# Splitting the causal mask of a decay product between its spare rows and an identity product, with constants, loads and two engines' orders rearranged

## Chip, cores and metric

One core of one Trainium2 chip. The metric is the device time of one execution in microseconds, median of several runs. Engines: PE (TensorE; its weight loads are shown apart as PEld), DVE (VectorE), ACT (ScalarE), POOL (GpSimd) and SP (SyncE, which here only issues DMAs).

## What is computed

A gated linear attention (2 batches, 8 heads, 768 steps, head size 40) feeds a dense mixture of four experts and then a gated product layer. All inputs are f32.

```python
for t in range(S):                       # attention
    m_new = np.maximum(f_gate[:, :, t] + m, i_gate[:, :, t])
    f_stab = np.exp(f_gate[:, :, t] + m - m_new); i_stab = np.exp(i_gate[:, :, t] - m_new)
    C = f_stab * C + i_stab * outer(vt, kt); n = f_stab * n + i_stab * kt
    y[:, :, t] = sigmoid(o_gate[:, :, t]) * (C @ qt) / max(abs(n @ qt), 1)
for e in range(4):                       # experts, x is y as 1536 x 320
    out += p[:, e:e+1] * (np.maximum(x @ w1[e], 0) @ w2[e])
result = ((out @ w_a) * (out @ w_b)) @ w_out
```

## The kernel before

**Attention in chunks.** Time is cut into 6 chunks of 128 steps; a chunk of one batch is a *unit*, 12 in all (`NU`), unit u being chunk u // 2 of batch u % 2. Inside a unit the recurrence becomes products: scores (`products`, L1519), times weights exp(log decay), times values (`outputs`, L1562), plus the part from the state (`from_state`, L1531), and an update of the state (`update`, L1545). The log weight of key step s and query step t is a sum of a term of s and a term of t, and minus 1e30 where s > t. `log_weights` makes it on PE for 4 heads at a time (q = 0, 1): first an identity product adds the mask (`identb` times `mask`, bf16, 512 columns, L1507), then the decay product (`dec_l` times `dec_r`, 66 rows, 512 columns, L1508) adds the rest. In `dec_l`, rows 0 to 15 and 32 to 47 hold the key term's high and low halves for the 16 heads, and rows 64 and 65 are ones; in `dec_r`, rows 0 to 63 pick the head and rows 64 and 65 hold the query term. ACT takes exp of both banks (`weights`, L602), DVE multiplies with the scores (`weigh`, L1063).

**Start.** POOL builds `identf`, `pick`, `ones`, `mask`, `identb` and parts of `dec_l` one after the other, counting them in `pool_const` and `mask_ready`. DVE clears the `qk` buffers and part of `dec_l`, then `first_logs` scans the gates of chunks 0 and 1 (from L1153 on) and makes the halves of the query terms, `lhi` (L1142) and `llo` (L1145). SP and ACT send these rows into `dec_r` by DMA, PE turns them into unit 0's log weights. Meanwhile a second scan (L1165) gives `m` for the rest, a DMA brings it back into another layout (`m_r`), and `rest_logs` makes the terms of chunks 2 to 5, which `load_dec_l` and `load_rows` bring by DMA into `dec_l` and `dec_r`. PE runs dummy products (`keep_busy`, L1481) while it has nothing else. SP's issues are written in a fixed order, each behind waits on semaphores.

**The layers.** 56 *groups* (`NG`): 8 plain ones, groups 8 to 31 for experts and 32 to 55 for the gated layer. From group 8 on a group has 7 products of 4 matmuls with 384 columns (L1619 to L1622) in two PSUM banks A and B, in a form with 7 instead of 8 block products. ACT and DVE combine them: ACT copies `keep_p1`, `keep_u2`, `keep_w` (L737, L745, L751), DVE makes `c11`, `c22`, `c12` (L1229, L1236, L1243), ACT rounds the result to the high half `hh` (L729), DVE makes the low half `hl` (L1214, L1220). Between a group's products PE does the second layer of the group before (L1700, 320 columns). Product 1 of a group waits till `c12` of the group before has left bank B (`b_free`), product 2 till `keep_p1` has left bank A.

**Groups 29, 30, 33 and 34** also turn the result of the layer before for the next (`turn_within`, 4 transposes each, L1472 and L1474): ACT replicates tails (`replicate`, L615), copies the turned tiles (`keep_turned`, L626) and rounds them (`x_high`, L641); DVE makes low halves (`x_low`, L1018, L1019) and differences (`x_sum`, L1038) for groups 32 and 36. New weights go through ACT (`high_a` L692, `high_s` L696), POOL (`low_a` L508, four `sums` L518 to L524, `low_s` L513); `high_s` of a tile can begin when POOL's four sums are done. What ACT and DVE do in these groups is written out by hand in `turning_expert`, `expert_group`, `turning_gated` and `gated_group`; engines work strictly in this order.

## Time and profile before

| what | us |
|---|---|
| median of 3 runs | 609.79 (609.6 to 610.05) |
| the profiled execution's own time | 610.64 |
| its span in the profile | 608.5 |
| PE busy | 599.8 (99%) |
| PE weight loads | 581.7 (96%) |
| DVE / ACT / POOL busy | 358.6 / 290.9 / 179.6 |
| granted TensorE clock, mean | 0.998 |

A timeline row gives start, length, engine, line and operation; a bracket at its end is the engine's idle time before it and what ended that. Ends of PE's matmuls are modelled, so an idle gap on PE shows best in the distance between starts.

### The profile page before, as it was taken

The numbers are of one execution on the slowest core, as the hardware profiler recorded it, in microseconds if no ns is written. First come the engines' busy times: TensorE is split into PE (matmuls) and PEld (weight loads), VectorE is DVE, ScalarE is ACT, GpSimd is POOL, SyncE is SP. The second block draws the span as 40 slices with busy tenths as digits, with TensorE's granted clock in tenths as the row PEclk, the third lists the DMA queues.
The fourth block names the chain that finished last, engine by engine and source line by source line (L and its number), as shares of the span: only waits on it lengthen the run. The fifth ranks groups of instructions, "written<-read, shape, count | busy, mean of one in ns | idle before, by whom it ended". The sixth has DMA issues, their size and how long they took to land.

```text
span 608.5 us, 10953 instructions
## 1 busy us (share of the span) xinstructions
PE 599.8 (99%) x4001; PEld 581.7 (96%) x4001; DVE 358.6 (59%) x706; ACT 290.9 (48%) x618; POOL 179.6 (30%) x246
## 2 busy tenths in 40 slices
PE   8999999999999999999999999999999999999997
PEld 7788999999999999999999999999899999999996
DVE  7767974454473444543535545477796665666555
ACT  5778745324443444443444434746744543444332
POOL 4466430015330134300334001332325521553000
PEclk9999999999999999999999999999999999999999
DMA  4756541003312021410022200112102410120011
GB/s 131 223 197 180 166 126 49 12 1 69 97 39 61 1 46 30 129 40 23 9 61 87 57 12 0 42 40 80 53 12 46 108 57 12 45 47 1 5 62 65
DMA packets 21028, 38.38 MB, mean 63 GB/s; under 512 B 3520, under 2 KB 11280, under 8 KB 20976
## 3 DMA queue, kind: packets, MB, share of 16 engines
q1 hardware_dynamic: 19040, 35.02, 20.4%
q10 hardware_dynamic: 1936, 2.67, 1.3%
q8 instruction: 32, 0.52, 0.4%
q14 instruction: 20, 0.16, 0.1%
HBM read 26.42 MB, written 1.97 MB: 47 GB/s over the span
## 4 chain that ended last, share of the span: by engine, by line
PE 92%; DVE 4%; DMA 1%; issue 1%; ACT 1%; SPq 0%; DVEq 0%; ACTq 0%
PE PS L1700 37%; PE PS L1619 12%; PE PS L1622 12%; PE PS L1620 11%; PE PS L1621 11%; PE PS L1562 2%; PE PS L1519 1%; PE PS L1531 1%; DMA dec_l<-alo_r 1%; PE PS L1472 1%; PE PS L1474 1%; PE PS L1507 1%; PE PS L1508 1%; PE PS L1545 0%; DMA dec_r<-llo 0%
## 5 line engine op out<-in xcount | busy, mean ns | idle before, releaser
L1700 PE MATMUL PS<-w2h,hh 128*128 128x320 f32 x528 | 164.9, 312 | 0.1
L1700 PE MATMUL PS<-w2l,hh 128*128 128x320 f32 x528 | 163.4, 309 | 0.0
L1700 PE MATMUL PS<-w2h,hl 128*128 128x320 f32 x528 | 163.2, 309 | 0.0
L1619 PE MATMUL PS<-xop,wop 128*128 128x384 f32 x400 | 138.9, 347 | 1.1 <-ACT p_s L737 0.6
L1622 PE MATMUL PS<-xop,wop 96*128 96x384 f32 x400 | 135.1, 338 | 0.0
L1620 PE MATMUL PS<-xop,wop 128*128 128x384 f32 x400 | 134.8, 337 | 0.0
L1621 PE MATMUL PS<-xop,wop 128*128 128x384 f32 x400 | 134.8, 337 | 0.0
L729 ACT ACTIVATE hh<-c_s 128x384 fp32r<-128x384 f32 x120 | 62.8, 523 | 100.4 <-DVE c_s L1243 27.9
L1700 PEld LDWEIGHTS PS<-w2h,hh 128*128 128x128 f32 x528 | 99.5, 189 | 0.8 <-DVE hl L1220 0.8
L1700 PEld LDWEIGHTS PS<-w2l,hh 128*128 128x128 f32 x528 | 99.7, 189 | 0.0
L1700 PEld LDWEIGHTS PS<-w2h,hl 128*128 128x128 f32 x528 | 99.4, 188 | 0.0
L1236 DVE TENSOR_TENSOR c_s<-PS,w_s 128x384 f32<-128x384 f32 x48 | 26.8, 557 | 99.8 <-ACT w_s L751 68.9
L1619 PEld LDWEIGHTS PS<-xop,wop 128*128 128x128 f32 x400 | 75.1, 188 | 6.9 <-issue 1.4
L1620 PEld LDWEIGHTS PS<-xop,wop 128*128 128x128 f32 x400 | 75.3, 188 | 0.0
L1622 PEld LDWEIGHTS PS<-xop,wop 96*128 96x128 f32 x400 | 75.2, 188 | 0.0
L1621 PEld LDWEIGHTS PS<-xop,wop 128*128 128x128 f32 x400 | 75.1, 188 | 0.0
L1214 DVE SCALAR_TENSOR_TENSOR hl<-PS,hh 128x384 fp32r<-128x384 f32 x56 | 31.1, 556 | 57.8 <-ACT hh L729 57.5
L513 POOL TENSOR_TENSOR wop<-s,wop 128x512 fp32r<-128x512 f32 x24 | 31.1, 1297 | 105.4 <-ACT wop L696 105.4
L729 ACT ACTIVATE hh<-PS 128x384 fp32r<-128x384 f32 x56 | 27.4, 489 | 71.8 <-PE PS L1700 38.2
L1214 DVE SCALAR_TENSOR_TENSOR hl<-c_s,hh 128x384 fp32r<-128x384 f32 x72 | 42.6, 592 | 27.9 <-ACT hh L729 27.9
L751 ACT ACTIVATE w_s<-PS 128x384 f32<-128x384 f32 x48 | 23.5, 490 | 64.3 <-PE PS L1622 64.2
L533 POOL TENSOR_TENSOR t1l<-t,t1h 128x384 fp32r<-128x384 f32 (+1 forms) x7 | 7.3, 1050 | 154.5 <-ACT t1h L703 154.5
(148 smaller groups left out, 811.3 us busy)
## 6 DMA issues: line engine op xcount, KB each, us to landing
s<-in_wt SPq DMA_DIRECT2D x24, 256.0 KB, 3.2
kvo<-in_tok SPq DMA_DIRECT2D x12, 480.0 KB, 3.8
wop<-t1h SPq DMA_DIRECT2D x48, 112.0 KB, 2.2
qk<-in_qk_t SPq DMA_DIRECT2D x24, 160.0 KB
s<-in_w SPq DMA_DIRECT2D x12, 320.0 KB, 3.0
wop<-t1l SPq DMA_DIRECT2D x24, 112.0 KB, 2.2
s<-in_w_out SPq DMA_DIRECT2D x12, 160.0 KB, 2.2
out_y<-acc SPq DMA_DIRECT2D x12, 160.0 KB, 1.9
```

What stands on the lines that cost most here:

```text
L513: nc.gpsimd.tensor_tensor(wop[p][:, 2, 3 * P:7 * P], s1[:, p, :], f32(wop[p][:, 0, 3 * P:7 * P]), ALU.subtract).then_inc(w_lo_s, 1)
L533: nc.gpsimd.tensor_tensor(t1l[:, to], t1[:, of], f32(t1h[:, to]), ALU.subtract).then_inc(t_lo, 1)
L729: nc.scalar.activation(hh[:, home(n, k), :], src, ACT.Relu if n < FIRST else ACT.Copy).then_inc(hh_ready, 1)
L751: nc.scalar.activation(w_s[:, :], PS[:, A_BANK, 0:HT], ACT.Copy).then_inc(w_kept, 1)
L1214: nc.vector.scalar_tensor_tensor(out=hl[:, home(n, k), :], in0=src, scalar=0.0, in1=f32(hh[:, home(n, k), :]), op0=ALU.max, op1=ALU.subtra ...
L1236: nc.vector.tensor_tensor(c22_s[:, :], PS[:, B_BANK, 0:HT], w_s[:, :], ALU.add).then_inc(c22_made, 1)
L1562: last = nc.tensor.matmul(PS[:, out_bank(u), D1 * h:D1 * (h + 1)], pt[b][q][:, p, :], vx[b][:, h, :], start=True, stop=True)
L1619: nc.tensor.matmul(to, ws[0], xs[0], start=opens, stop=False, skip_group_check=True)
L1620: nc.tensor.matmul(to, ws[0], xs[2], start=False, stop=False, skip_group_check=True)
L1621: nc.tensor.matmul(to, ws[2], xs[0], start=False, stop=False, skip_group_check=True)
L1622: return nc.tensor.matmul(to, ws[1][0:96, :], xs[1][0:96, :], start=False, stop=closes, skip_group_check=True)
L1700: got = nc.tensor.matmul(bank, left, (w2l if part == 1 else w2h)[p][:, f, :], start=opens and part == 0, stop=closes and part == 2)
```

## The change

Four things. **Mask**: rows 66 to 127 of `dec_r` now hold minus 1e30 on a diagonal over columns 0 to 61 of each head, and the same rows of `dec_l` a staircase of ones, so that the decay product (now 128 rows) masks these 62 columns itself; the identity product covers only the other 66 (264 columns for 4 heads) and comes second. **Constants**: POOL sets all of `dec_l` (one fill, one select over 768 columns) and clears `qk1`; `first_logs` waits for this select; ACT writes two more pieces per `dec_r`. **Loads**: unit 1's `qk` goes behind the first rows, `dec_l` of chunk 2 (units 4 and 5) ahead of unit 2's `kvo` and unit 3's `qk`; `llo` is made before `li` is reduced. **Orders**: ACT and DVE in groups 29 to 35 (`prepare_early`, which held `high_s` and `high_a` of two tiles, is split into `prepare_parted_sums` and `prepare_parted`).

```diff
@@ POOL, start @@
-            nc.gpsimd.memset(f32(dec_l[64:PICKED, :, :]), 1.0).then_inc(pool_const, 1)
+            nc.gpsimd.memset(f32(dec_l[:, :, :]), 1.0).then_inc(pool_const, 1)
             pool.wait_ge(pool_const, 5)
+            nc.gpsimd.affine_select(out=dec_l[:, :, :], in_=dec_l[:, :, :], compare_op=ALU.is_ge, fill=0.0, base=PICKED - 1,
+                                    pattern=[[0, NC], [1, P]], channel_multiplier=-1).then_inc(pool_const, 1)
...
-            nc.gpsimd.memset(f32(dec_l[0:64, 2:NC, :]), 0.0).then_inc(pool_const, 1)
+            nc.gpsimd.memset(qk[1][:, :, :, :], 0.0).then_inc(pool_const, 1)
@@ ACT, def pick_heads @@
+                for at, of, by in ((0, PICKED, NEG), (STEPS, 0, 0.0)):
+                    cols = STEPS if of else P - STEPS
+                    nc.scalar.activation(dec_r[b][64:P, :, at:at + cols], identf[64:P, of:of + cols].unsqueeze(1).to_broadcast([64, H, cols]),
+                                         ACT.Copy, scale=by).then_inc(picked, 1)
@@ DVE, def logs_of @@
-                nc.vector.tensor_tensor(li, li, lsum, ALU.subtract).then_inc(done, 1)
                 dve.wait_ge(done, n + 6)
                 nc.vector.tensor_tensor(llo, lsum, f32(lhi), ALU.subtract).then_inc(rows_ready, 1)
+                nc.vector.tensor_tensor(li, li, lsum, ALU.subtract).then_inc(done, 1)
@@ DVE, def first_logs @@
-                dve.wait_ge(dve_const, 2)
-                dve.wait_ge(pool_const, 4)
+                dve.wait_ge(dve_const, 1)
+                dve.wait_ge(pool_const, 6)
@@ SP @@
-            sp.wait_ge(qk_zero, 2)
-            load_qk(1)
             load_first_high_row(0)
             load_first_high_row(1)
+            sp.wait_ge(pool_const, 11)
+            load_qk(1)
...
             load_qk(2)
+            load_dec_l(2)
             load_kvo(2)
-            load_qk(3)
-            sp.dma_start(pe_w[:, :, :].rearrange("p e u -> p (e u)"), probs).then_inc(probs_in, 16)
-            load_dec_l(2)
@@ PE, def log_weights @@
-                    nc.tensor.matmul(PS[:, DEC + q, :], identb[:, :], mask[:, :, :].rearrange("s p t -> s (p t)"), start=True, stop=False)
-                    nc.tensor.matmul(PS[:, DEC + q, :], dec_l[0:PICKED, c, :], dec_r[b][0:PICKED, q:H:2, :], start=False, stop=True).then_inc(dec_done, 1)
+                    to = PS[:, DEC + q, :]
+                    nc.tensor.matmul(to, dec_l[:, c, :], dec_r[b][:, q:H:2, :], start=True, stop=False, skip_group_check=True)
+                    nc.tensor.matmul(to.rearrange("s (p t) -> s p t", p=NP)[:, :, STEPS:P], identb[:, :], mask[:, :, :],
+                                     start=False, stop=True, skip_group_check=True).then_inc(dec_done, 1)
@@ PE @@
-            keep_busy(14)
+            keep_busy(13)
             products(0)
-            keep_busy(4)
+            keep_busy(3)
@@ ACT, def turning_expert @@
                 keep_u2(n)
-                if b2 is not None:
-                    x_high(b2, 0)
+                prepare_weights(n)
                 high_c11(n)
                 keep_w(n)
                 keep_turn(n, 1)
                 replicate_late(b1, 3)
                 if b2 is not None:
-                    x_high(b2, 1)
+                    x_high(b2, 0)
                 high_c21(n)
                 keep_turn(n, 2)
                 if b2 is not None:
+                    x_high(b2, 1)
                     x_high(b2, 2)
-                prepare_weights(n)
                 high_c22(n)
@@ ACT, def turning_gated @@
                 replicate_late(b2, 5)
+                prepare_parted_sums(n)
                 keep_w(n)
                 keep_turn(n, 1)
-                prepare_early(n)
-                replicate_late(b1, 3)
                 keep_turn(n, 2)
                 high_product(n, 0)
+                prepare_parted(n)
+                replicate_late(b1, 3)
@@ DVE, def expert_group @@
                 low_relu(n, 2, c22_s[:, :])
+                make_c12(n)
                 if b3 is not None:
                     x_low(b3, 4)
-                make_c12(n)
-                if b3 is not None:
                     x_sum(b3, 3)
@@ DVE, def turning_expert @@
                     x_low(b2, 0)
-                    x_low(b2, 1)
                 low_relu(n, 1, PS[:, A_BANK, 0:HT])
                 make_c22(n)
+                if b2 is not None:
+                    x_low(b2, 1)
@@ DVE, def gated_group @@
-                if b3 is not None:
-                    w2_lows(n - 1)
                 make_c12(n)
@@ DVE, def turning_gated @@
                 make_c22(n)
-                if b1 is not None:
-                    x_low(b1, 0)
                 if b2 is not None:
                     x_low(b2, 2)
                 make_c12(n)
                 low_product(n, 0, c11_s[:, :])
                 make_ab2(n)
                 if b1 is not None:
+                    x_low(b1, 0)
                     x_low(b1, 1)
+                if b2 is not None:
+                    w2_lows(n)
```

Where it shows in the orders of the engines:

POOL at the start of the program, before and then now (`pool_const` counts the constants; 6 is the select on `dec_l`).

```order
L458 MEMSET ones 128x128 [waits pool_const]
L459 MEMSET mask 128x512
L462 AFFINE_SELECT mask<-mask 128x512 [waits mask_ready]
L464 CAST identb<-identf 128x128
L466 MEMSET dec_l 2x768 [waits mask_ready]
L469 MEMSET vx0 128x8 [waits pool_const]
L470 MEMSET state0 128x328
```

```order
L458 MEMSET ones 128x128 [waits pool_const]
L459 MEMSET mask 128x264
L462 AFFINE_SELECT mask<-mask 128x264 [waits mask_ready]
L464 CAST identb<-identf 128x128
L465 MEMSET dec_l 128x768
L468 AFFINE_SELECT dec_l<-dec_l 128x768 [waits pool_const]
L471 MEMSET vx0 128x8
```

What `dec_l` needs is now two instructions over 768 columns and stands ahead of the states; DVE's first scan, which waited for `ones`, now waits for the second of them, as the next two pieces show (DVE, first instructions, before and now).

```order
L1118 MEMSET m 16x1
L1119 MEMSET dec_l 64x256
L1120 MEMSET qk0 128x1024
L1121 MEMSET qk1 128x1024
L1153 SCALAR_TENSOR_TENSOR m<-gate,m 16x256 [waits gates_in,pool_const,dve_const]
```

```order
L1126 MEMSET m 16x1
L1127 MEMSET qk0 128x1024
L1159 SCALAR_TENSOR_TENSOR m<-gate,m 16x256 [waits gates_in,pool_const,dve_const]
```

ACT in group 30 and the start of group 31, before and now (`wop1<-s1 128x384` is `high_a`, `wop1<-s1 128x512` is `high_s` of the same tile, `p1_s` is `keep_p1`).

```order
L745 ACTIVATE u2_s<-PS 128x384 [waits c12_made,prod_done]
L641 ACTIVATE xop0<-raw 128x2x384 [waits prod_done,raw_ready]
L729 ACTIVATE hh<-c11_s 128x384 [waits l2_done,c11_made]
L751 ACTIVATE w_s<-PS 128x384 [waits c22_made,prod_done]
L626 ACTIVATE raw<-PS 128x2x2x128 [waits x_lo,xt_done]
L641 ACTIVATE xop0<-raw 128x2x384 [waits prod_done,raw_ready]
L729 ACTIVATE hh<-PS 128x384 [waits l2_done,prod_done]
L626 ACTIVATE raw<-PS 128x2x2x128 [waits x_lo,xt_done]
L641 ACTIVATE xop0<-raw 128x2x384 [waits prod_done,raw_ready]
L692 ACTIVATE wop1<-s1 128x384 [waits prod_done,w_in1]
L729 ACTIVATE hh<-c22_s 128x384 [waits l2_done,c22_made]
L696 ACTIVATE wop1<-s1 128x512 [waits w_sum]
L729 ACTIVATE hh<-c12_s 128x384 [waits l2_done,c12_made]
L737 ACTIVATE p1_s<-PS 128x384 [waits c11_made,prod_done]
```

```order
L750 ACTIVATE u2_s<-PS 128x384 [waits c12_made,prod_done]
L697 ACTIVATE wop1<-s1 128x384 [waits prod_done,w_in1]
L734 ACTIVATE hh<-c11_s 128x384 [waits l2_done,c11_made]
L756 ACTIVATE w_s<-PS 128x384 [waits c22_made,prod_done]
L631 ACTIVATE raw<-PS 128x2x2x128 [waits x_lo,xt_done]
L646 ACTIVATE xop0<-raw 128x2x384 [waits prod_done,raw_ready]
L734 ACTIVATE hh<-PS 128x384 [waits l2_done,prod_done]
L631 ACTIVATE raw<-PS 128x2x2x128 [waits x_lo,xt_done]
L646 ACTIVATE xop0<-raw 128x2x384 [waits prod_done,raw_ready] x2
L734 ACTIVATE hh<-c22_s 128x384 [waits l2_done,c22_made]
L701 ACTIVATE wop1<-s1 128x512 [waits w_sum]
L734 ACTIVATE hh<-c12_s 128x384 [waits l2_done,c12_made]
L742 ACTIVATE p1_s<-PS 128x384 [waits c11_made,prod_done]
```

`high_a`, which starts POOL's chain, moved from the place ahead of `c22`'s rounding to right behind `u2_s`; `high_s`, which ends it, stayed.

DVE in group 31, before and now (`xop0` is `x_low(2, 4)`).

```order
L1214 SCALAR_TENSOR_TENSOR hl<-PS,hh 128x384 [waits hh_ready]
L1214 SCALAR_TENSOR_TENSOR hl<-c22_s,hh 128x384 [waits hh_ready]
L1018 TENSOR_TENSOR xop0<-raw,xop0 128x384 [waits x_hi]
L1019 TENSOR_TENSOR xop0<-raw,xop0 32x384
L1243 TENSOR_TENSOR c12_s<-PS,u2_s 128x384 [waits u2_kept,prod_done]
```

```order
L1220 SCALAR_TENSOR_TENSOR hl<-PS,hh 128x384 [waits hh_ready]
L1220 SCALAR_TENSOR_TENSOR hl<-c22_s,hh 128x384 [waits hh_ready]
L1249 TENSOR_TENSOR c12_s<-PS,u2_s 128x384 [waits u2_kept,prod_done]
L1026 TENSOR_TENSOR xop0<-raw,xop0 128x384 [waits x_hi]
L1027 TENSOR_TENSOR xop0<-raw,xop0 32x384
```

`c12` no longer stands behind the two instructions of `x_low`.

## Rows read from the trace of the kernel before

**Rows 1.** Who waited for whom, engine PE, whole span: us, times, longest
```profile
PE PS L1507 <- DMA dec_l<-alo_r: 1.0, 1, 1.0
```

**Rows 2.** Chain that ended last, 0 to 90 us: start us, us, what
```profile
3.23 0.63 DVE m L1153
...
7.22 2.39 DMA dec_r<-llo
...
16.99 6.50 DMA dec_l<-alo_r
```

**Rows 3.** Timeline of POOL: start us, us, engine, line, operation, count
```profile
1.17 0.29 POOL L453 TENSOR_SCALAR_AFFINE_SELECT identf<-identf 128x128 f32<-128x128 f32 x1 [0.24 <-POOL identf L451]
...
2.64 0.63 POOL L462 TENSOR_SCALAR_AFFINE_SELECT mask<-mask 128x512 bf16<-128x512 bf16 x1
3.22 0.71 POOL L464 CAST identb<-identf 128x128 bf16<-128x128 f32 x1
3.99 0.73 POOL L466 MEMSET dec_l<- 2x768 f32 x1
```

**Rows 4.** Timeline of DVE, the logs of the later chunks begin
```profile
12.41 0.28 DVE L1125 TENSOR_TENSOR lf_r<-gate_r,m_r 80x128 f32<-80x128 f32 x1
```

**Rows 5.** Timeline of PE, start of the program
```profile
2.08 5.20 PE L1481 MATMUL PS<-ones 128*128 128x128 f32 x28 [2.08 <-POOL ones L458]
...
8.30 1.16 PE L1481 MATMUL PS<-ones 128*128 128x128 f32 x8
```

**Rows 6.** Timeline of PE, log weights of unit 6
```profile
35.44 0.39 PE L1507 MATMUL PS<-mask,identb 128*128 128x512 bf16 x1
...
35.90 0.39 PE L1507 MATMUL PS<-mask,identb 128*128 128x512 bf16 x1
```

**Rows 7.** Timeline of PE weight loads, the same place
```profile
35.43 0.10 PEld L1507 LDWEIGHTS PS<-mask,identb 128*128 128x128 bf16 x1
35.44 0.20 PEld L1508 LDWEIGHTS PS<-dec_r,dec_l 66*128 66x128 f32 x1
```

**Rows 8.** Timeline of DVE, unit 7's numerators
```profile
58.11 0.50 DVE L1099 TENSOR_TENSOR num<-PS,inter_s 128x328 f32<-128x328 f32 x1 [0.48 <-PE PS L1562]
```

**Rows 9.** Windows by group: length, busy PE PEld DVE ACT POOL, clock, DMA
```profile
354.24:364.42 10.18, 10.18 (x66) 10.18 (x65) 4.36 (x9) 3.43 (x7) 0.00 (x0) 1.00 0.06 18
...
398.20:409.24 11.04, 10.48 (x67) 10.21 (x65) 8.77 (x14) 5.62 (x11) 3.05 (x4) 1.00 0.14 33
409.24:419.95 10.71, 10.65 (x66) 10.19 (x65) 9.19 (x17) 5.26 (x13) 3.12 (x5) 1.00 0.40 121
419.95:429.54 9.59, 9.30 (x60) 8.84 (x59) 5.86 (x13) 7.98 (x20) 3.54 (x5) 1.00 0.17 46
429.54:439.26 9.72, 9.58 (x59) 8.74 (x59) 7.57 (x14) 7.04 (x15) 2.41 (x3) 1.00 0.17 44
...
447.18:455.62 8.44, 8.37 (x48) 7.52 (x47) 8.15 (x18) 3.66 (x7) 1.86 (x3) 1.00 0.07 20
455.62:463.29 7.67, 7.67 (x48) 7.56 (x47) 5.20 (x11) 3.46 (x7) 3.00 (x6) 1.00 0.01 2
```

**Rows 10.** Timeline of ACT, groups 30 and 31
```profile
395.56 0.51 ACT L692 ACTIVATE wop<-s 128x384 fp32r<-128x384 f32 x1
...
400.17 0.63 ACT L696 ACTIVATE wop<-s 128x512 fp32r<-128x512 f32 x1 [3.15 <-POOL s L524]
```

**Rows 11.** Timeline of DVE, groups 31, 34 and 35
```profile
408.88 0.55 DVE L1018 TENSOR_TENSOR xop<-raw,xop 128x384 fp32r<-128x384 f32 x1
...
410.04 0.56 DVE L1243 TENSOR_TENSOR c_s<-PS,u_s 128x384 f32<-128x384 f32 x1
...
433.20 0.56 DVE L1229 TENSOR_TENSOR c_s<-PS,p_s 128x384 f32<-128x384 f32 x1 [0.54 <-PE PS L1622]
...
446.26 1.20 DVE L1053 TENSOR_TENSOR w2l<-s,w2h 128x320 fp32r<-128x320 f32 x1
```

**Rows 12.** Timeline of ACT, group 33
```profile
426.40 0.58 ACT L626 ACTIVATE raw<-PS 128x512 f32<-128x512 f32 x1
```

37 lines of the change are left out of this document (18 added, 19 removed).

## The prediction

> **What bounds the kernel now.** I read the page first: PE is busy 599.8 of 608.5 us (the table above), so only what shortens PE's own work, or a place where PE stands, can change the time much. The list of PE's waits names one long one in the attention part, 1.0 us for a DMA into `dec_l` [rows 1]; it is short because ends of matmuls are modelled, so I looked for the rest in the lengths of the groups. In the chain that ended last the reader sees how the start hangs together: DVE's first scan at 3.23, the DMA of the first rows at 7.22 (landed 2.39 later), and the DMA of `dec_l` for chunk 2, which took 6.50 us from 16.99 [rows 2]. In the windows by group a quiet expert group takes 10.18 us and a quiet gated one 7.67, with PE full [rows 9]. Groups 31 and 32 take 11.04 and 10.71, so PE stood 0.86 and 0.53 us in them. Groups 33 and 34 have 28 matmuls of 384 columns, 18 of 320 and 12 of a transpose; by the quiet groups (36 of 320 in one, 18 in the other, so 18 of them make 10.18 - 7.67 = 2.51) and 12 transposes at about 0.11 they should take 7.67 + 1.3 = 9.0, and take 9.59 and 9.72: 0.6 and 0.7 lost. Group 36 takes 8.44, 0.77 lost. Together about 3.5 us of standing, and the change rearranges just these groups.
>
> **The change, part by part.**
>
> *Mask products.* Each of 12 units has two identity products of 512 columns, now 264. Start to start, an identity product and its decay product take 35.90 - 35.44 = 0.46 us for 1024 columns [rows 6], so 248 columns are 0.11 us, 0.22 per unit, if nothing else decides. But the first product of each pair is now the decay product, whose f32 weights take 0.20 us to load against 0.10 for the bf16 identity [rows 7], and this load stands right behind a wait, while `dec_l`'s used to lie under the identity's columns. That can give back 0.10 per unit at one exposed load, 0.20 at two. I take 0.10 saved per unit (0 to 0.22), since for one of the two loads 264 columns of the pair before are there to cover it. The Trainium skill (TensorE: Matmul & The Clock Gate, LDWEIGHTS and Weight-path perf modes) says that a load goes by its columns at 1.2 GHz, 107 ns for 128, and that only types other than f32 load faster. By it a streamed 264 columns would just cover a load, and a unit would save some 0.1 us more; by the same rule the swap of a fast first load for a slow one speaks against the change. Rows 7 agree that f32 loads take twice as long as bf16 ones.
>
> *Which units count.* Units 0 to 2 wait for rows, exp and logs, so nothing there. From unit 3's log weights to unit 9's PE is the bound. Behind that DVE is: it still had 0.48 us idle before unit 7's numerators [rows 8], and none afterwards, so the savings of units 10 and 11 wait for DVE. Seven units give 0.7 (0 to 1.5).
>
> *The wait for `dec_l` of chunk 2.* Its DMAs were issued behind 480 KB of `kvo` (128 x 960 f32 in the code) and 320 KB of `qk` and took 6.50 us; now they go ahead of these. PE's 1.0 us [rows 1] goes. What is behind them now: `kvo` of unit 2, rows of unit 4 and `qk` of unit 3 are issued 3 to 5 us later. PE needs `qk` of unit 3 about 1 us after unit 4's log weights, and by my count it lands about 1 us before that. So -1.0 (bounds -1.0 and, if that `qk` is late by 1, 0).
>
> *The start.* DVE's first scan ran at 3.23 [rows 2], when the gates had landed. Now it waits for POOL's select on all of `dec_l`. POOL's old times: select of 128 columns 0.29, of 512 0.63, the cast 0.71, a fill of 768 columns 0.73 [rows 3]. The new mask is half as wide, so its fill ends about 0.26 earlier and its select starts at 2.38 and takes 0.29 + 136 x 0.34/384 = 0.41: 2.79. Cast to 3.50 (3.0 if the 0.71 was a collision with DVE, whose engine now is idle), fill of `dec_l` to 4.2, 0.15 for the wait, select of 768 columns by the same slope 0.86: 5.2. The scan moves by 1.5 to 2.1; I take 1.8, between the two casts. The upper bound is 2.9, if a select on f32 costs twice the bf16 one; the lower is 0.8, if cast and fill overlap. With `llo` ahead of `li` the first rows leave 0.3 earlier than that, at 7.22 - 0.3 + 1.8 = 8.7. Everything that follows from the first scan moves: the second scan, the return of `m` and the logs of the later chunks, which began at 12.41 [rows 4], now at 14.2. ACT's additional pieces of `dec_r` (4 of about 500 columns, 0.6 us each) end near 6.6 and are covered till 8.7. `qk1`'s fill on POOL ends near 7.5, its load is issued behind the rows near 10.2 and should land near 13.5, before PE asks at 14: nothing. At unit 4, PE would have been free 1.0 us before its old start: 1.8 late, minus 1.0, minus 0.1 of unit 3.
>
> *Sum of the attention part*: +1.8 - 1.0 - 0.7 = +0.1 (bounds: +0.8 - 1.0 - 1.5 = -1.7 and +2.9).
>
> *Group 31.* ACT stood 3.15 us at 400.17 for POOL's sums, with `c12`'s rounding and `keep_p1` queued behind it [rows 10], and PE behind that for bank A. `high_a` of the tile, at 395.56, is 4.6 us ahead of it, so ACT waits as long as POOL's chain takes. Now `high_a` goes behind `keep_u2`, some 5 us earlier, and the sums are there before ACT asks. The 0.86 goes. Next in line is DVE's `c11` of group 31, with 1 us to spare.
>
> *Group 32.* DVE made `c12` of group 31 at 410.04, behind `x_low` from 408.88 (1.16 us) [rows 11], and behind a chain that had itself begun late through group 31's stall. PE's first wait (bank B) and its second (bank A, through ACT) hang on it: 0.53. With `c12` first and the chain on time, both go: -0.5.
>
> *Group 33.* ACT copied the third turned tile at 426.40 [rows 12], behind `high_s`, `high_a` and a replication (1.5 us), and PE stood about 0.5 for it. Now `high_s` lies in an idle stretch before and the other two behind: -0.5.
>
> *Group 34.* `c12` of group 33 also stood behind an `x_low` of 1.16 and gated PE's first turn and the low half behind it; of the 0.7 lost here I take back 0.5. But both `x_low` (2.3 us) now stand in a row ahead of `c11` of group 34, which had 0.54 idle before it at 433.20 [rows 11]: 1.16 more work into 0.54 of room makes it about 0.6 late, and PE's second turn waits for it, with at most a few matmuls in hand: +0.3 (0 to 0.6).
>
> *Groups 35 and 36.* DVE is without idle time from 437 to 447 there. The low half of `w2` took 1.20 at 446.26 [rows 11], just ahead of the `c12` for which PE then stood; moved to the end of group 34 it should take its usual 0.5. DVE's chain in 36 gains about 0.7, minus what it inherits; PE gets 0.4 of it, since product 5 of group 36 waits for the last `x_low`.
>
> *Sum of the groups*: -0.85 - 0.5 - 0.5 - 0.5 + 0.3 - 0.4 = -2.4. Bounds: -3.2 if all standing goes, -0.9 if only group 31's does.
>
> **Total**: +0.1 - 2.4 = -2.3. Against the profiled execution's own 610.64 (span 608.5 and 2.1 around it) that is 608.3; this execution lies 0.85 above the median of 609.79, so in medians **607.5**. A measurement of this kernel can tell some 0.2% (1.2 us) from no change.
>
> **Rivals.**
>
> 1. *The start is not late.* If the select and the cast cost little, or the waits behind the scan have slack, the delay is 0.8, and if the narrow identity products save the full 0.22, the attention part gives -1.7: 609.8 - 1.7 - 2.4 = 605.7. For it: the cast's 0.71 looks long for 128 columns. Against: POOL works strictly in order and the scan is the head of the chain.
> 2. *The standing in the groups moves on instead of going.* DVE is over 80% busy in groups 31, 32 and 36 (8.77 of 11.04, 9.19 of 10.71, 8.15 of 8.44 [rows 9]); if it stays the bound there, only group 31's 0.86 goes: 609.8 + 0.1 - 0.9 = 609.0.
> 3. *`qk` of unit 3 is the new wait.* 320 KB issued about 5 us later than before, behind `kvo`: 0.8 us given back, 608.3. So the loads would not do what they are ordered for.
> 4. *The late start costs PE its clock (slower than before).* Between the last dummy product, near 8.7, and the first rows, near 11.2, PE has nothing. At the start of the program PE needed 5.20 us for 28 passes, later 1.16 for 8 [rows 5]: at the later pace 28 would be 4.1, so the slow start cost 1.1. If PE falls back in the gap and pays this again, and the scan is 2.9 late instead of 1.8, and the groups give only half: 609.8 + (0.1 + 1.1 + 1.1) - 1.2 = 610.9. It decides once the scan runs later than about 6 us into the span. Against it: the granted clock stays 1.00 in the rows of the groups, through gaps of up to 0.9 us [rows 9], and much of the loss would lie in units that wait for logs anyway. The Trainium skill (TensorE: Matmul & The Clock Gate, HAM oscillation) has the rule that PE-idle gaps throttle the clock to half and that it is won back by sustained work; no gap of this length is in the trace of before.
>
> **How the numbers follow.** The forecast 607.5 has a chance of 0.62 (its own range 606.3 to 608.6), rival 1 0.12, rival 2 0.12, rival 3 0.08, rival 4 0.06. The range from 605.6 to 609.2 leaves out rival 4 and the tails of the first two. Faster by over 0.2% is under 608.6: 0.62 x 0.9, all of rival 1, two thirds of rival 3, little of rival 2, together 0.75. Slower by over 0.2% is part of rival 4: 0.05. The rest, 0.20, is no change.
>
> **What the profile of the changed kernel should show.** DVE's first scan near 5.0, behind a wait for POOL; the first rows near 8.7; no wait of PE on a DMA into `dec_l`; unit 4's log weights near 24.6 instead of 23.96; 0.10 less from one unit to the next between 30 and 53 us. The length of group 31 at 10.2, 32 at 10.2, 33 at 9.1, 34 near 9.5, 36 near 8.0, all others unchanged. The forecast is wrong if the scan is at 3.2 or past 6, if a unit saves nothing or 0.2, if the granted clock shows a fall near 10 us, or if groups 32 to 36 keep their lengths.

## The result and the profile after

The changed kernel takes **615.85 us** (median of 6 runs, 611.2 to 620.93) against 609.92 for the kernel before, run beside it. The ratio is 1.0082, 95% interval 1.0044 to 1.0120 (it leaves out runs over 1.5% above the fastest of their kernel; medians here take all runs). Forecast were 607.5 and a range of 605.6 to 609.2. Of the rivals, the fourth, to which I gave 0.06, is what happened, though not as it was priced.

The six runs differ in one thing, their mean granted clock: 611.2 us at 0.996, 614.61 at 0.989, 615.35 at 0.989, 616.34 and 616.73 at 0.985, 620.93 at 0.978. The profile below is that of the first, which lost least (span 609.3), so it shows the mechanism but not its usual size.

PE's waits of the first 90 us, in the same view as [rows 1]. Columns: total, times, longest.

```profile
PE PS L1513 <- DMA dec_r<-llo: 3.0, 2, 1.7
...
PE PS L1526 <- DMA qk<-in_qk_t: 0.2, 1, 0.2
```

The wait for `dec_l` [rows 1] is gone, as forecast. In its place stand two waits for the first rows, 3.0 us together where the kernel before had one of 0.4, and a new one for `qk`. The chain up to 40 us, against [rows 2]:

```profile
3.90 0.86 POOL dec_l L468
4.87 0.75 DVE m L1159
...
10.40 3.19 DMA dec_r<-llo
...
28.76 4.50 DMA qk<-in_qk_t
```

The scan runs at 4.87 behind POOL's select, where 5.0 was forecast. The chain then does not go through unit 0's rows but through the second DMA, that of unit 1's low row, which took 3.19 from 10.40. PE's timeline there:

```profile
8.88 0.94 PE L1486 MATMUL PS<-ones 128*128 128x128 f32 x6
11.20 0.46 PE L1513 MATMUL PS<-dec_r,dec_l 128*128 128x512 f32 x1 [1.38 <-DMA dec_r<-llo]
...
13.96 0.48 PE L1513 MATMUL PS<-dec_r,dec_l 128*128 128x512 f32 x1 [1.66 <-DMA dec_r<-llo]
...
14.32 0.75 PE L1513 MATMUL PS<-dec_r,dec_l 128*128 128x512 f32 x1
```

PE stands 1.38 us ahead of unit 0's log weights and 1.66 ahead of unit 1's. Right behind, the product that took 0.47 takes 0.75: the clock has fallen. Stretches of 4 us from 8 us on (length, busy time of PE, PEld, DVE, ACT and POOL, granted clock, DMA share, GB/s):

```profile
8.00:12.00 4.00, 2.62 (x26) 1.99 (x24) 3.14 (x7) 0.00 (x0) 0.00 (x0) 1.00 0.13 19
12.00:16.00 4.00, 2.34 (x11) 1.51 (x11) 1.29 (x2) 2.88 (x7) 0.72 (x1) 0.79 0.74 211
16.00:20.00 4.00, 4.00 (x35) 3.63 (x33) 3.74 (x12) 2.21 (x6) 1.58 (x2) 0.78 0.27 85
```

The first two of these in the kernel before:

```profile
8.00:12.00 4.00, 3.45 (x25) 2.20 (x22) 2.14 (x4) 1.49 (x5) 0.17 (x1) 1.00 0.32 69
12.00:16.00 4.00, 3.90 (x38) 3.32 (x36) 3.86 (x11) 3.27 (x9) 2.21 (x3) 1.00 0.49 150
```

In 12:16 of the changed kernel the DMA engines are 0.74 busy: `qk` of unit 1 and `kvo` travel beside the small transfers. The return of `m` in the profile's DMA issues from 7 to 20 us (KB, us to landing), in the changed kernel,

```profile
m_r<-m SPq DMA_DIRECT2D x1, 40.0 KB, 3.2
m_r<-m ACTq DMA_DIRECT2D x1, 40.0 KB, 4.6
```

and in the kernel before:

```profile
m_r<-m SPq DMA_DIRECT2D x1, 40.0 KB, 2.2
m_r<-m ACTq DMA_DIRECT2D x1, 40.0 KB, 2.5
```

So the logs of the later chunks begin at 16.02, 3.6 later than in [rows 4], where the scan is 1.64 later. From unit 6 on, unit follows unit in 5.65 us (log weights of units 6 and 7), by start to start, against 5.75 before:

```profile
38.03 0.50 PE L1513 MATMUL PS<-dec_r,dec_l 128*128 128x512 f32 x1
...
43.68 0.50 PE L1513 MATMUL PS<-dec_r,dec_l 128*128 128x512 f32 x1
```

Groups 31, 32, 33, 34 and 36, against [rows 9]:

```profile
400.81:410.99 10.18, 10.18 (x66) 10.18 (x65) 8.98 (x15) 5.20 (x10) 1.04 (x1) 1.00 0.15 35
410.99:421.17 10.18, 10.18 (x66) 10.18 (x65) 9.39 (x17) 5.37 (x13) 3.26 (x5) 1.00 0.44 127
421.17:430.36 9.19, 9.19 (x61) 8.83 (x59) 6.04 (x11) 7.30 (x17) 2.89 (x4) 1.00 0.17 48
430.36:440.63 10.27, 9.71 (x59) 8.70 (x59) 8.91 (x15) 7.84 (x18) 2.83 (x4) 1.00 0.15 42
448.55:456.72 8.17, 8.14 (x49) 7.54 (x47) 7.87 (x17) 3.61 (x7) 1.97 (x4) 1.00 0.00 0
```

Group 31 gives 0.86, 32 gives 0.53, 33 gives 0.40, 36 gives 0.27, and 34 takes 0.55 more. Group 29, of which the prediction says nothing, takes 0.28 more (12.18 for 11.90). The sum by group starts: group 8 starts at 162.92 instead of 160.61 (+2.31), the groups give about 1.2 back, and another 0.3 comes back behind group 36, which leaves the 0.8 between the two spans. The execution shown thus loses only 0.8 against the profile of before; the other five lose more, with a lower clock.

### The profile page after: what moved, and what is told of

Same layout as the page of the kernel before. It is cut to its first block, busy times and chain, and to the rows that moved or that the text cites. A ratio compares the mean times of both kernels' runs of the same rounds, so it can differ in the third digit from the quotient of the medians.

```text
span 609.3 us, 10949 instructions
## 1 busy us (share of the span) xinstructions
PE 599.1 (98%) x3997; PEld 583.6 (96%) x3997; DVE 360.0 (59%) x704; ACT 293.9 (48%) x622; POOL 179.2 (29%) x247
## 4 chain that ended last, share of the span: by engine, by line
PE 93%; DVE 4%; DMA 1%; issue 1%; POOL 1%; ACT 0%; ACTq 0%; DVEq 0%; POOLq 0%; SPq 0%
PE PS L1707 37%; PE PS L1626 12%; PE PS L1629 11%; PE PS L1627 11%; PE PS L1628 11%; PE PS L1569 3%; PE PS L1526 2%; PE PS L1538 1%; PE PS L1513 1%; PE PS L1477 1%; PE PS L1479 1%; DMA qk<-in_qk_t 1%; DMA dec_r<-llo 1%; PE PS L1552 1%; DVE xop L1027 0%
## 5 line engine op out<-in xcount | busy, mean ns | idle before, releaser
L1220 DVE SCALAR_TENSOR_TENSOR hl<-c_s,hh 128x384 fp32r<-128x384 f32 x72 | 42.1, 585 | 24.6 <-ACT hh L734 24.6
```

Source lines behind the costliest of these rows:

```text
L1220: nc.vector.scalar_tensor_tensor(out=hl[:, home(n, k), :], in0=src, scalar=0.0, in1=f32(hh[:, home(n, k), :]), op0=ALU.max, op1=ALU.subtra ...
```

## The experiments

The theories, as the expectations name them. **A**: the late scan makes PE stand, and standing brings the clock down. **B**: the order of SP's loads costs the time. **C**, formed after the first eight kernels: within that order it is `qk` of unit 1, now behind the first rows. Each kernel was run 6 to 12 times; the kernel before took 610.2 to 610.6 beside them. The changed kernel itself was not run again beside them, so that comparisons with its 615.85 go over two sets of runs, in which the kernel before took 609.92 and 610.2 to 610.6.

### The scan early again

```diff
-                dve.wait_ge(pool_const, 6)
+                dve.wait_ge(pool_const, 4)
...
+                dve.wait_ge(pool_const, 6)
                 nc.vector.tensor_copy(dec_l[0:BH, 0:2, :], first_two).then_inc(logs0, 1)
```

> The changed kernel, but DVE's first scan waits for POOL only up to the fill of ones again; the wait for the select of dec_l stands just ahead of the first rounding into dec_l. Theory A (the late scan costs PE its clock and delays the start): the scan is back at about 3.2, the first rows leave near 7.0, the granted clock stays at 1.0 from about 6 us on, group 8 starts near 160.9 (162.92 in the changed kernel, 160.61 before), and the time is 608.5 to 609.5, the same in every run within 0.5. Rival B (the order of SP's loads costs the time, through qk of a later unit and the second row of unit 1): the scan is early, but PE waits for qk between units 3 and 5 as long as in the changed kernel, group 8 starts at 162 or later, and the time is 611 or more.

**615.86 us** (613.52 to 619.91 in 6 runs), mean clocks 0.980 to 0.992, no better than the changed kernel. Theory A in this form is refuted, and the reason has two parts. First, the scan is back at 3.17, but the first product comes at 10.57, since DVE's operations that now run beside POOL's are stretched:

```profile
3.94 1.10 DVE L1131 TENSOR_TENSOR wgt<-gate,m 16x256 f32<-16x256 f32 x1
...
5.74 0.76 DVE L1136 TENSOR_SCALAR wgt<-wgt 16x256 f32<-16x256 f32 x1
```

In the changed kernel they take 0.41 and 0.28. POOL's select of `dec_l` runs from 3.90 to 4.76 and its fill of `qk` from 5.41 to 6.36, and the two DVE operations end 0.28 and 0.14 behind these. The Trainium skill (SBUF — State Buffer, SBUF: two separate sides) has GpSimd and some of DVE's operations share a pair of ports by an exclusive lock, the loser blocked for the whole instruction; the trace agrees for these two. It does not hold for any pair: the two operations on two tensors that follow at 4.97 and 5.30 ran beside POOL's fills of the states and took 0.41 and 0.40. Second, the three dummies end early (8.85), so PE stands 1.73 and then 1.08 us, and the clock falls at 12.30. PE's standing, then, and not the scan's hour, is what these two kernels share.

### Dummies where PE stood

```diff
-            keep_busy(3)
+            keep_busy(11)
             log_weights(0)
             turn_first_logs()
+            keep_busy(5)
             log_weights(1)
```

> The changed kernel, scan still late, with 8 more dummy products ahead of unit 0's log weights and 5 ahead of unit 1's, which fill the two stretches in which PE stood 2.3 and 1.7 us. Theory A in its half on the clock: the granted clock no longer falls near 14 us, and the spread from run to run (spans from 609.3 to 614.8) closes; what is left is the delay itself, so 610.5 to 611.3. Rival B: clock and spread have another cause than the standing; the clock falls all the same, and the runs lie between 611 and 617.

**612.04** (610.09 to 618.81), 3.8 less than the changed kernel and 0.7 above the 610.5 to 611.3 expected. Nine of twelve runs have a mean clock of 0.996 to 1.0; three, at 616.6 or more, have 0.986 to 0.988. The profile fell on one of these:

```profile
16.00:20.00 4.00, 2.63 (x20) 2.14 (x20) 3.76 (x12) 2.73 (x7) 1.67 (x2) 1.00 0.29 88
20.00:24.00 4.00, 3.76 (x28) 2.70 (x30) 3.47 (x11) 2.74 (x8) 0.12 (x1) 0.51 0.38 126
```

PE now stands one place further on, 1.60 us ahead of the turning of the later logs, which wait for `m`. This one gap was enough here: the clock fell near 20.1 and was back near 37.1. So a third gap remained, and it was reason to fill that as well:

### More dummies

```diff
-            keep_busy(1)
+            keep_busy(4)
...
                 if u == 1:
+                    keep_busy(4)
                     log_weights(2)
+                    keep_busy(5)
                     turn_rest_logs()
```

> The changed kernel with dummies ahead of unit 0's (8 more) and unit 1's (5) log weights, as in the run before this, and further ones ahead of unit 1's products (3 more), unit 2's log weights (4) and the turning of the later logs (5), where PE still stood 1.6 us. Theory A: no run has the clock at a half any longer, all runs lie within 1.5 us of each other, at 609.8 to 611. If the clock still falls in a quarter of the runs, as in the run with fewer dummies (3 of 12 above 616), standing is not what brings it down.

**612.39** (612.16 to 612.71), all clocks 0.999 or 1.0. The median is 1.4 above the 611 expected, but the spread of 9.7 us in the changed kernel has shrunk to 0.55. Feeding PE removes the falls altogether; what it can't remove is the delay, to which surplus dummies add.

### SP's loads in the old order, PE fed

```diff
             load_kvo(0)
+            sp.wait_ge(pool_const, 11)
+            load_qk(1)
             load_first_high_row(0)
             load_first_high_row(1)
-            sp.wait_ge(pool_const, 11)
-            load_qk(1)
...
-            load_dec_l(2)
             load_kvo(2)
+            load_qk(3)
...
+            load_dec_l(2)
```

> The changed kernel with the first set of dummies (8 and 5) and SP's loads in the old order, with the late scan kept. Against the run with these dummies alone (610.1 at best, 612.0 median): rival B has the loads cost some 1 us (PE's wait for qk of unit 4, the later second row of unit 1), so 609.0 at best here; theory A has them at nothing or a gain of up to 1 us, which is lost here, so 610 to 611 at best.

**609.72** (609.21 to 610.48), clocks 0.999 to 1.0 in all twelve. It differs from the first set of dummies (612.04) in the loads alone, and PE no longer stands at the turning of the logs:

```profile
16.00:20.00 4.00, 3.96 (x41) 3.07 (x40) 3.90 (x10) 3.37 (x9) 1.62 (x2) 1.00 0.62 188
```

The order of the loads costs 2.3 us in the median and 0.9 between the best runs; theory B had 609.0 for the best, 1.1 less. Which load it is, the next pair tells.

### `qk` of unit 1 ahead again, and with PE fed

The edit is the first half of the one above; the second kernel adds the 8 and 5 dummies.

> The changed kernel with one thing undone: qk of unit 1 is loaded ahead of the first rows again. The late scan, the dec_l load ahead, the 13 and 3 dummies stay. Theory C (the 320 KB of qk behind the first rows are what hurts: they share the DMA engines with the second row of unit 1 and with m on its way back, 3.19 and 4.6 us instead of 2.4 and 2.5, and PE stands a second and a third time): unit 1's log weights follow unit 0's as in the kernel with a late scan alone (12.3, not 13.96), the rest of the logs start near 14.0 instead of 16.0, the clock falls seldom and briefly, and the time is 609.5 to 611. Theory A in its first form (the late scan is what hurts): 613 or more, as the changed kernel.

> The changed kernel with qk of unit 1 loaded first and the 8 and 5 dummies; dec_l of chunk 2 stays ahead of the bulk. It differs from the run with all loads in the old order (609.72) only in dec_l and the qk and kvo behind it. If these cost nothing: 609.2 to 609.8, and PE's 0.36 at unit 4's log weights goes. If qk of unit 4 comes late (it took its data at 33.07 in the changed kernel, PE standing 0.16 to 0.3): 609.9 to 610.5.

Unfed **610.67** (609.43 to 619.23), four of twelve above 613; unit 1's log weights at 12.78 instead of 13.96 (12.3 expected; the clock was at a half there in this profile, the longest of the twelve). Fed **609.68** (609.21 to 610.37), which equals the 609.72 of the old order. So `qk` of unit 1 is the load that hurts (5.2 of 5.9 us come back with this one edit), and `dec_l` ahead of the bulk is neither gain nor loss.

The two profiles also show how it hurts. ACT's second issue of a low row begins at 10.3 to 10.4 in both, and SP and ACT issue their halves of `m_r` at 11.31 to 11.32 in both; what differs is the landing. The return of `m` from 7 to 20 us, with `qk` of unit 1 ahead (3.2 and 4.6 in the changed kernel):

```profile
m_r<-m SPq DMA_DIRECT2D x1, 40.0 KB, 2.2
m_r<-m ACTq DMA_DIRECT2D x1, 40.0 KB, 2.7
```

The later logs begin at 14.07 instead of 16.02. This profile also has the longest single gap of all: PE stands 2.49 us ahead of unit 0's log weights, hardly (0.37) ahead of unit 1's, and the clock is at a half from 12.1 to 36.0.

In the fed kernel PE has no wait for `dec_l`, and stands for `qk` of unit 4 instead. PE's waits there, 20 to 36 us:

```profile
PE PS L1526 <- DMA qk<-in_qk_t: 0.8, 1, 0.8
```

### The loads from unit 2 on, on the kernel before

Group orders of the changed kernel, and the load order from unit 2 on.

> The kernel before with the group orders of the changed one and its order of SP's loads from unit 2 on (dec_l of chunk 2 ahead of kvo of unit 2, qk of each unit behind the rows of the next). Group orders alone gave 608.9. Rival B (the loads cost time: qk of unit 3 or 4 lands late, PE stands for it): 609.5 or more, a wait of PE on qk of 0.5 us or more between 20 and 34 us. Theory A (the loads are harmless or a gain, as the prediction had it): PE's 1.0 for dec_l goes, group 8 starts 0.5 to 1.0 earlier than with the group orders alone (159.4), 607.9 to 608.5; the clock stays at 1.0.

**609.10** (608.24 to 619.54), against 608.91 for the group orders alone. PE had no wait of 0.5 for `qk`, nor the gain that A expected: these loads neither gain nor lose, which agrees with the pair above. In this profile (609.78, mean clock 0.997) PE stood 1.30 us ahead of unit 0's log weights, and the clock was at a half for 3.4 us behind it.

### The late scan, and `qk` behind the rows, one at a time and together

```diff
# late scan, in the kernel before
-                dve.wait_ge(pool_const, 4)
+                dve.wait_ge(pool_const, 5)
# qk behind, in the kernel before
-            sp.wait_ge(qk_zero, 2)
-            load_qk(1)
             load_first_high_row(0)
             load_first_high_row(1)
+            sp.wait_ge(qk_zero, 2)
+            load_qk(1)
```

> The kernel before with one number changed: DVE's first scan waits for POOL's fill of rows 64 and 65 of dec_l, so that it runs near 4.8 instead of 3.2. Nothing else moves. Theory A: this alone makes PE stand about 2 us ahead of unit 0's log weights and 1 to 2 more in units 1 and 2, the granted clock falls to a half in some or all runs between 10 and 20 us, and the time is 1.5 to 6 above the kernel before, with a spread. Rival B (the late scan costs its 1.6 us or less, and the clock and the spread come from the reordered loads): 609.8 to 611.4, all runs within 0.6 of each other, no fall of the clock.

> The kernel before with one thing changed: qk of unit 1 is loaded behind the two first high rows. Scan at 3.2, everything else as before. Theory C: the second row of unit 1 lands later by 1 us or more, m_r too, PE stands ahead of unit 1's and unit 2's log weights, the clock falls in a good part of the runs, and the time is 611 to 616 with a spread. Theory A: this costs 0.5 or less, the clock stays at 1.0, 609.8 to 610.8.

> The kernel before with two edits: the scan waits for POOL's fill of rows 64 and 65 (late scan, alone 611.6), and qk of unit 1 is loaded behind the first high rows (alone 612.4). If these two are the whole loss: the changed kernel's 615.85 plus the 1.3 that its group orders give back, so 615.5 to 618, no run at a mean clock of 1.0, with a spread of several us. If they only add up: 613.8 (609.8 + 1.6 + 2.2), and the rest of the loss lies in another part of the change. If they cover each other: 612 to 613.

Late scan: **611.60** (610.64 to 630.61); the scan ran at 4.40. Its profile was taken at 611.93, mean clock 0.997. PE stood 1.56 us once, ahead of unit 0's log weights, and the clock was at a half for 3.4 us from 12.5 on, in which PE had hardly any idle time:

```profile
12.00:16.00 4.00, 3.84 (x22) 2.92 (x23) 3.61 (x11) 3.59 (x10) 1.53 (x2) 0.57 0.53 149
16.00:20.00 4.00, 4.00 (x48) 3.38 (x44) 3.21 (x9) 2.30 (x7) 0.88 (x1) 1.00 0.73 215
```

`qk` behind: **612.40** (610.51 to 630.40). Both together: **621.56** (612.64 to 632.60; 615.5 to 618 expected), clocks 0.962 to 0.997, none at 1.0. Added up, the two would be 613.8; together they cost 11. By the ratios to the kernel before, too, the pair (1.0114, 1.0078 to 1.0151) costs about twice the sum of the two (1.0021 and 1.0034). The profile of the pair fell on one of its longest runs:

```profile
12.00:16.00 4.00, 2.42 (x8) 1.50 (x7) 2.50 (x7) 1.95 (x6) 0.72 (x1) 0.50 0.67 198
16.00:20.00 4.00, 4.00 (x26) 3.69 (x26) 3.38 (x10) 2.63 (x7) 1.71 (x2) 0.50 0.37 104
...
40.00:48.00 8.00, 8.00 (x51) 6.67 (x52) 2.69 (x8) 4.57 (x10) 2.89 (x4) 0.50 0.42 138
```

PE stood 1.90 and 1.58 us, ahead of the log weights of unit 0 and of unit 1. The clock fell at 11.87, between the two gaps, and came back at 59.66; from 16 us on PE reads as busy all that time, and at half the clock.

### The late scan, with PE fed

The late scan in the kernel before, with `keep_busy(9)` for `keep_busy(4)` ahead of unit 0 and one more dummy ahead of unit 1.

> The kernel before with the late scan (4.4 instead of 3.2) and dummies against the standing that it causes: 5 more ahead of unit 0's log weights, 1 ahead of unit 1's. The late scan alone gave 611.6, with mean clocks of 0.997 and 0.999 in nine runs and 0.989 or less in three. If standing is what brings the clock down: mean clock 1.0 or 0.999 in all runs, nothing above 612, median 610.6 to 611.2. If the clock falls from something else in the first microseconds: again runs above 615.

**610.88** (610.71 to 611.52), clocks 0.999 to 1.0 in all eleven. The scan is just as late as in the unfed kernel, of which a quarter of the runs lay at 617 or more. This is the cleanest pair: what brings the clock down is that PE stands. The delay itself costs 0.25 us between the medians (610.63 beside it, with falls of its own) and 1.1 between the best runs (609.64 and 610.71).

### The groups' orders alone

The kernel before with the ACT and DVE orders of groups 29 to 35.

> The kernel before with only the orders of groups 29 to 36 of the changed one (ACT's and DVE's). Theory A: group lengths change as they did in the changed kernel (31 by -0.85, 32 by -0.5, 33 by -0.4, 34 by +0.5, 36 by -0.3), so the time is 1.3 to 1.8 below the kernel before, 608.0 to 608.5. Rival C: the gain of the groups in the changed kernel was there because PE came to them later, so that the other engines had got ahead; then the gain here is under 0.8.

**608.91** (607.99 to 629.59 in 8 runs), ratio 0.9972 (0.9961 to 0.9983). Groups: 31 by -0.86, 32 by -0.53, 33 by -0.38, 34 by +0.57, 36 by -0.28. The lengths are those of theory A, and the gain of 1.3 does not depend on PE's being late; the median is 0.4 above the 608.0 to 608.5 expected.

### The old start with the split, and a version meant to beat both

The first: the changed kernel with the scan early, both fills of `qk` on DVE, the old load order and 14 and 4 dummies. The second cuts POOL's select too and moves one `x_low`; the third adds 2 dummies ahead of unit 0 and 1 ahead of unit 1.

```diff
-            nc.gpsimd.memset(f32(dec_l[:, :, :]), 1.0).then_inc(pool_const, 1)
+            nc.gpsimd.memset(f32(dec_l[:, 0:2, :]), 1.0).then_inc(pool_const, 1)
...
+            pool.wait_ge(m_ready, 1)
+            nc.gpsimd.memset(f32(dec_l[:, 2:NC, :]), 1.0).then_inc(pool_const, 1)
...
                 make_c11(n)
+                if b2 is not None:
+                    x_low(b2, 1)
...
                     x_low(b1, 0)
-                    x_low(b1, 1)
```

> The changed kernel with the start and the loads of the kernel before: the scan waits only for the fill of ones, DVE fills both qk buffers, SP's loads stand in the old order, 14 and 4 dummies. What is left of the change are the split mask product and the orders of the groups. Theory A (what costs the time is PE standing between 8 and 20 us, which brings the clock to a half): the first rows leave near 7.9, since DVE still collides with POOL's select, PE stands about 1 us instead of 0.4 ahead of unit 0, the clock falls in few runs or none, and the time is 607.8 to 609.0. Rival D (the split product itself or the longer filling of dec_r disturbs the start): PE stands 1.5 us or more ahead of units 0 or 1, the clock falls in most runs, and the time is 611 or more.

> A version meant to beat both: the old start and loads, the split mask product, POOL's fill and select of dec_l cut in two (chunks 0 and 1 early, the other four once DVE has made m, when it stands), and the x_low of tile 1 moved from the end of group 33 to behind c11 of group 34. Against the run with the old start and the split (608.9, group 34 10.27, scan chain stretched by POOL, first row product at 10.60): if POOL's select was what stretched DVE (1.10 for 0.41), the first product comes near 10.0; if x_low ahead of c11 was what made PE stand 0.58, group 34 takes 9.6 to 9.8. Together 607.4 to 608.2; the clock at 1.0. If DVE is stretched all the same and the standing moves to another wait of group 34 or 35, 608.6 to 609.

> The version meant to beat both with 2 more dummies ahead of unit 0's log weights and 1 ahead of unit 1's. Over the profiled runs so far the clock first rose to 1.0 between 4.9 and 8.3 us; where it rises early the dummies end early and PE stands. If the spread of that version (607.7 to 615.2) comes from that, the extra dummies close it: all runs within 1 us, 607.9 to 608.9, since in runs with a late rise they push unit 0 back by up to 0.8. If the spread stays (some runs above 612), the fall of the clock has another cause than this gap.

First: **608.92** (608.53 to 609.43); first product at 10.60, group 34 10.27. The split itself does no harm. Second: **608.90** (607.66 to 615.20). Both mechanisms hold: DVE's operation beside POOL takes 0.44 for 1.10, the first product comes at 10.17, and group 34 takes 9.69. But the median is 0.7 above the 607.4 to 608.2 expected: four runs lie at 607.7 to 608.2 with a clock of 1.0, the others at 608.5 and above with less. Third: **608.14** (607.60 to 609.87 in 7 runs), ratio 0.9965 (0.9951 to 0.9978), the fastest kernel of the study. The large losses are gone; one run with a clock of 0.996 (609.87) is left, which was not expected.

### `x_low` moved in the kernel before

> The kernel before with the new group orders, and x_low of tile 1 moved from the end of group 33 to behind c11 of group 34. Group 34 takes 9.7 instead of 10.27 to 10.30 as in the best version (9.69), the others as with the group orders alone (608.9): 608.2 to 608.6.

Group 34 takes 9.72, as expected; the time is **609.00** (608.28 to 618.79 in 8 runs), no less than the 608.91 without it. In this profile group 8 starts 1.43 later than in that one, in two steps: PE's first log weights are 0.71 late, since the clock first rose later, and PE then waits 0.7 for `dec_l`, which in the other profile it does not. From group 8 on this profile is 0.5 shorter. The gain is there in the groups and can't be seen in the median: the start varies by more from run to run.

### ACT's program shifted

> The kernel before with the group orders and four small extra copies on ACT at the start (parts of what it writes anyway), so that ACT's program is shifted by as many instructions as the split mask product shifts it, with nothing else of it. Group 29 took 11.95 in the three kernels without the split and 12.18 to 12.23 in the six with it, ACT starting hh 0.37 instead of 0.09 behind the signal. If that comes from where ACT's instructions stand in its program: 12.2 here. If it comes from the split itself (other tiles, other state of the queues): 11.95.

Group 29 took 12.23, as in the kernels with the split. The time was **610.23** (608.78 to 611.14 in 8 runs), 1.3 above the group orders alone: five of the eight have a mean clock of 0.996 or 0.997 and take 610.1 or more, the other three 608.8 to 609.0, and the profile is one of the latter. What the copies do to the start of the five is not shown. The row of ACT in question, first with the group orders alone, then with the four small copies in addition:

```profile
380.90 0.49 ACT L729 ACTIVATE hh<-PS 128x384 fp32r<-128x384 f32 x1 [0.66 <-PE PS L1702]
```

```profile
381.70 0.49 ACT L733 ACTIVATE hh<-PS 128x384 fp32r<-128x384 f32 x1 [0.94 <-PE PS L1706]
```

ACT starts 0.28 later behind the same signal. So the 0.28 of group 29 comes from where ACT's instructions lie in its program. In the shifted kernel the DMA records have an instruction packet 0.6 to 0.7 us behind that start, and none within 2 us of it in the other. The Trainium skill (Runtime: NRT & Kernel Launch, Instruction fetch mechanics) says that an engine's program comes in blocks whose crossing is mostly hidden; that this is a crossing that isn't hidden is argued from the packet, not shown.

## Why the prediction was wrong, point by point

- **Mask products**: right, 0.10 less per unit (5.65 for 5.75), and nearly right for the whole: from unit 3's log weights to group 8 the kernel with the group orders alone takes 142.02 and the version meant to beat both, which adds the split and keeps the order of the loads, 141.43, so 0.6 for the 0.7 forecast. From unit 11's log weights on the second is 0.2 longer, as the prediction had it for units 10 and 11. The 107 ns on which its "some 0.1 us more" rests is not what an f32 load takes here: 0.20 [rows 7].
- **The wait for `dec_l`**: between the two profiles the wait went and its 1.0 came back (log weights 3.74 late at unit 3, 2.54 at unit 4). In the medians no gain came: 609.68 for 609.72 with PE fed, 609.10 for 608.91 with the group orders on the kernel before. The reason is in the other profiles. Of the profiles of twelve kernels with `dec_l` in its old place only three show PE waiting for it: the kernel before (1.0), `qk` behind (0.8) and `x_low` moved (0.7). So -1.0 was the price in one execution, a slow one, from which the prediction then took off another 0.85 for being above the median; that the two are in part the same microsecond is likely, not shown. The prediction saw the next in line, `qk`, but for unit 3 and "about 1 us before"; it was unit 4's, and PE stood for it 0.2 in the changed kernel and 0.8 in the fed one with `qk` of unit 1 ahead. That is rival 3's mechanism, one unit on.
- **The start, first half**: scan 4.87 for 5.0, first rows 8.71 for 8.7. Right.
- **The start, second half: the step that failed.** "`qk1`'s fill on POOL ends near 7.5, its load is issued behind the rows near 10.2 and should land near 13.5, before PE asks at 14: nothing." The load was issued at 10.30 and did land in time for its own reader. I costed it by that reader alone. It shared the DMA engines with what was on the path: unit 1's low row (landed 3.19 after its issue) and `m` (4.6 for 2.5). Everything behind was not 1.8 late but 2.7 at unit 1 and 3.6 at the later logs, and unit 4's log weights came at 26.50 where 24.6 was forecast. Undoing it alone gives 5.2 us back.
- **The clock**: rival 4 named the mechanism and had three sizes wrong. The scan didn't have to pass 6 us: 4.87 was enough, and 4.40 in the late-scan kernel. The price wasn't the 1.1 of a slow start: the clock stayed at a half for 3.4 us in the changed kernel's profile, 13.7 in the one with an early scan and 47.8 in the longest. (The 1.1 was itself too small: 8 passes take 1.16 and 6 take 0.94, so a pass is 0.11, and the 28 passes of 5.20 lost about 2.) And the argument against it, the full clock in the groups "through gaps of up to 0.9 us", set gaps that were shorter (the longest that the trace lists there is 0.56, ahead of the product at 401.65) against ones of 1.4 and 1.7; one gap of 1.56 was already enough in the late-scan kernel. The Trainium skill's rule (TensorE: Matmul & The Clock Gate, HAM oscillation) on PE-idle gaps bore on just this; the trace agrees with its fall to half. It does not agree that sustained work wins the clock back soon: in the longest profile PE read as busy from 16 us on, and the clock was back at 59.66.
- **Groups**: 31 and 32 exact (-0.86, -0.53), 33 -0.40 for -0.5, 36 -0.27 for -0.4. **Group 34** is +0.55 for -0.2: the +0.3 for both `x_low` ahead of `c11` was the right mechanism at twice the size, and the -0.5 for `c12` wasn't there: with one of the two behind `c11`, group 34 took 9.69 and 9.72, no less than the 9.72 of before. These rows of the changed kernel show it, PE then DVE:

```profile
435.36 0.33 PE L1477 MATMUL PS<-identf,acc 128*128 128x128 f32 x1 [0.56 <-DVE c_s L1235]
```

```profile
433.57 0.56 DVE L1026 TENSOR_TENSOR xop<-raw,xop 128x384 fp32r<-128x384 f32 x1
434.16 0.55 DVE L1027 TENSOR_TENSOR xop<-raw,xop 32x384 fp32r<-32x384 f32 x1
434.75 0.56 DVE L1235 TENSOR_TENSOR c_s<-PS,p_s 128x384 f32<-128x384 f32 x1
```

  Group 29's +0.28 was in no step. The groups' sum was -1.2 for -2.4.
- **What the whole comes to**: with PE fed and `qk` of unit 1 ahead, the changed kernel takes 609.68 beside 610.63 for the kernel before, ratio 0.9982 (0.9963 to 1.0001). So without the failed step and the fall of the clock it is worth about 1 us, which the interval does not quite tell from nothing, where 2.3 were forecast; the groups alone fell 1.2 short.

Open are how long the clock stays down, which was 3.4, 13.7, 17.1, 23.9 or 47.8 us with no cause seen in the traces, why one gap brings it down in some runs of a kernel and not in others, and the rest of the spread in the best version. The size of the loss, 5.9 us in the median, is mostly this duration: the execution that kept its clock best took 611.2.

## What to carry over

Cost a moved transfer by what travels beside it, not by whether its own reader gets it in time: 320 KB set going just as the small transfers on the path leave can cost more than any wait that it spares. At the start of a program, where PE waits for a chain of small steps, count PE's gaps one after another. A single one of 1.3 to 2.5 us already put the clock at risk here, and two close together did so in every run. Dummy products that just fill them cost next to nothing (610.71 at best with, 610.64 without, in the late-scan pair), while twelve more in the changed kernel took away the spread and cost 2.1 between the best runs (610.09 and 612.16). Compare clocks run by run before believing a profile: here the profiled run was the best of six.

## What the runs showed of the hardware

- Gaps of 1.4 and 1.7 us in PE, with 1.1 us of work between them, were followed by a fall of the granted clock from 2.4 to 1.2 GHz at 14.36 us in the changed kernel. One gap was enough in the profiles of the late scan alone (1.56 us, mean clock 0.997), of the first dummies (1.60) and of `qk` of unit 1 ahead (2.49). With the late scan five of twelve runs had a mean clock of 0.999, four 0.997 and three 0.989 or less; with two gaps, in the pair of edits, none of ten had above 0.997. Where dummies filled the gaps, all 46 runs of four kernels had 0.999 or 1.0.
- Once down, the clock stayed at 1.2 GHz for 3.4 us in the changed kernel, 13.7 with the scan early and 47.8 in the pair of edits, though PE reads as busy throughout from 16 us on in all three.
- The moment at which the first products of PE went over to twice the pace (from 4 or 5 of them in half a microsecond to 7) varied from 4.9 to 8.3 us over the profiles, and with it the moment at which the same dummies ended; the clock column reads 1.00 there already, so that it is no help before the first fall. The Trainium skill (TensorE: Matmul & The Clock Gate, What's actually happening) says that this moment varies from run to run, by half a microsecond either way; the profiles agree that it varies, and spread over 3.4 us.
- A select on POOL over 768 columns stretched a DVE operation on two tensors from 0.41 to 1.10, and a fill of 1024 columns one on a tensor and a scalar from 0.28 to 0.76. Operations on two tensors kept their 0.41 beside a fill (5.64, in the changed kernel).
- A transfer of 40 KB that was issued at the same time took 4.6 us to land with 320 KB of `qk` issued just ahead of it, and 2.7 without.
- Four more instructions at the start of ACT's program made another instruction, 380 us later, start 0.28 later.
